# Attention on one core: a threshold on GpSimd, sums of even groups put elsewhere, weight parts made earlier

## The reference

```python
scores = (q @ k.T) / sqrt(64)
thresh = max(scores, -1) - tau
scores = where(scores >= thresh, scores, -1e9)
attn = exp(scores - max(scores, -1))
attn = attn / (sum(attn, -1) + 1e-9)
x = attn @ v                                   # then heads side by side: 2304 x 512
h = x @ w_in; sm = softmax(h); solu = h * sm
ln = (solu - mean) / sqrt(var + 1e-6) * g_ln; x = ln @ w_out
h = x @ w_in2; out = softplus(h) @ w_out2
```

## Time and profile before

| | |
|---|---|
| median of 3 runs | 910.83 us |
| the profiled execution | 911.15 us, span from first to last instruction 909.4 us |
| PE, DVE busy share of the span | 96%, 84% |
| ACT, POOL busy share of the span | 55%, 48% |
| chain that ended last | DVE 53%, PE 35%, issue 8% |
| attention | from 5.4 us (first score product) to about 254 us (last mask) |
| mean granted TensorE clock | 0.994 of full speed |

### The profile page before, as it was taken

The page is one execution under the profiler, slowest core; times in us unless marked ns, Lnnn a source line. Parts: engine busy times, 40 slices in busy tenths (PEclk is TensorE's granted clock), DMA queues, the critical chain, the costliest instruction groups (busy, mean ns, idle before and its releaser), DMA issues.

```text
span 909.4 us, 16546 instructions
## 1 busy us (share of the span) xinstructions
PE 869.7 (96%) x6104; PEld 726.3 (80%) x6104; DVE 762.1 (84%) x1376; ACT 501.7 (55%) x936; POOL 433.4 (48%) x449
## 2 busy tenths in 40 slices
PE   6899999999989999999998998999999999999997
PEld 4566666666667889889898897999989999899995
DVE  6999999999929754835641999999999999999997
ACT  4777877888846442433442564545545455455543
POOL 3445444447617612313311565565555556556563
PEclk9999999999999999999999899999999999999999
DMA  6813431342100000000002610000000000000000
GB/s 163 217 32 80 102 97 37 80 105 75 48 25 23 24 1 1 1 1 1 1 12 88 197 30 0 36 1 1 35 1 1 35 1 1 35 0 0 35 0 35
DMA packets 29496, 37.65 MB, mean 41 GB/s; under 512 B 3696, under 2 KB 17520, under 8 KB 29424
## 3 DMA queue, kind: packets, MB, share of 16 engines
q1 hardware_dynamic: 29024, 36.42, 14.5%
q10 hardware_dynamic: 400, 0.30, 0.1%
HBM read 31.98 MB, written 4.72 MB: 40 GB/s over the span
## 4 chain that ended last, share of the span: by engine, by line
DVE 53%; PE 35%; issue 8%; POOL 1%; ACT 1%; DMA 0%; ACTq 0%; DVEq 0%; POOLq 0%
DVE g L850 12%; PE y_ps L1044 11%; DVE ntop L710 8%; PE s_ps L942 7%; DVE g_hi L854 7%; DVE g L840 5%; PE h_ps L911 5%; DVE g_lo L856 5%; DVE g L843 5%; PE o_ps L982 4%; PE f_ps L1101 3%; PE m_ps L1020 2%; DVE x_lo L705 2%; DVE solu L807 1%; DVE st_top L793 1%
## 5 line engine op out<-in xcount | busy, mean ns | idle before, releaser
L451 POOL TENSOR_TENSOR w_lo<-w_raw,w_hi 128x512 fp32r<-128x512 f32 x96 | 129.6, 1351 | 163.6 <-ACT w_hi L632 163.6
L412 POOL TENSOR_SCALAR kept<-kept,inv 128x576 f32<-128x576 f32 x144 | 106.1, 756 | 117.9 <-DVE inv L742 117.8
L511 ACT ACTIVATE expd<-s_ps,ntop 128x576 f32<-128x576 f32 x144 | 106.3, 741 | 51.7 <-DVE ntop L710 51.7
L1020 PE MATMUL m_ps<-y_hi,w_lo 128*128 128x384 f32 x384 | 131.4, 342 | 0.0
L648 ACT ACTIVATE l<-u 128x384 f32<-128x384 f32 x96 | 50.4, 525 | 145.8 <-POOL u L459 145.8
L1020 PE MATMUL m_ps<-y_lo,w_hi 128*128 128x384 f32 x384 | 130.3, 339 | 0.0
L1020 PE MATMUL m_ps<-y_hi,w_hi 128*128 128x384 f32 x384 | 129.2, 336 | 0.0
L459 POOL TENSOR_TENSOR u<-z,consts 128x384 f32<-128x384 f32 x96 | 108.2, 1127 | 41.8 <-ACT z L641 41.7
L850 DVE TENSOR_TENSOR g<-g,l 128x384 f32<-128x384 f32 x96 | 125.7, 1309 | 2.7
L1101 PE MATMUL f_ps<-w_hi,g_hi 128*128 128x512 f32 x288 | 115.4, 401 | 8.9 <-DVE g_lo L856 8.9
L710 DVE TENSOR_REDUCE ntop<-s_ps 128x1 f32<-128x576 f32 x144 | 107.5, 757 | 14.2 <-PE s_ps L942 6.8
(11 more groups left out here) (87 smaller groups left out, 1815.1 us busy)
## 6 DMA issues: line engine op xcount, KB each, us to landing
q_sb<-q_t SPq DMA_DIRECT2D x28, 288.0 KB, 5.1
v_sb<-v_main SPq DMA_DIRECT2D x16, 256.0 KB, 3.2
stage<-w_in SPq DMA_DIRECT2D x16, 256.0 KB, 2.7
w_raw<-w_out SPq DMA_DIRECT2D x8, 512.0 KB, 4.8
out<-o_sb SPq DMA_DIRECT2D x5, 768.0 KB, 3.5
k_sb<-k_t SPq DMA_DIRECT2D x21, 144.0 KB, 4.4
stage<-w_in SPq DMA_DIRECT2D x4, 512.0 KB, 8.9
stage<-w_out SPq DMA_DIRECT2D x4, 512.0 KB, 3.7
```

The source lines that it names most:

```text
L412: nc.gpsimd.tensor_scalar(kept[:, tile % RING, :], kept[:, tile % RING, :], inv[:, group % 2, k:k + 1], 1.0, ALU.mult, ALU.mult).then_inc( ...
L451: nc.gpsimd.tensor_tensor(w4[1][:, n % 2, :], w4_raw[:, n % F2, :], f32(w4[0][:, n % 2, :]), ALU.subtract).then_inc(w4lo_made, 1)
L511: nc.scalar.activation(expd[:, tile % 2, :].rearrange("p (a b) -> p a b", a=2), s_ps[tile % 2][:, :, 0:HALF], ACT.Exp, bias=ntop[:, tile % ...
L1020: last = nc.tensor.matmul(m_ps[n % 4][:, 0:GC], w[:, k, (n % F2) * P:(n % F2 + 1) * P], y[odd][:, k, :], start=(k == 0 and m == 0), stop=( ...
```

## The change

GpSimd gets a loop over doubles instead of groups. In double u it makes the threshold of tile b (`make_threshold_b`), then the probabilities of the groups that ended in double u - 1, in the eighth double of a unit the key scalings of the next two pairs, and in doubles 28, 31, 37 and 40 two low parts each of the first matrix. VectorE makes the threshold of tile a alone; the semaphore is split in two. `raise_sums` of an even group moves from between the two maxima of the next double to behind the mask of b in the same double; odd groups stay. ScalarE's high parts go from doubles 54 to 61 to doubles 24 to 34, two in three.

```diff
+W1_LOW = (28, 31, 37, 40)
-        thresh_made = sem("thresh_made")
+        thresh_a, thresh_b = sem("thresh_a"), sem("thresh_b")
+        def complete(u):
+            return [group for group in range(GROUPS) if (GROUP * group + GROUP - 1) // 2 == u]
...
-            for group in range(GROUPS):
+            def make_threshold_b(u):
+                pool.wait_ge(top_made, 2 * u + 2)
+                col = slice((2 * u + 1) % 4, (2 * u + 1) % 4 + 1)
+                nc.gpsimd.tensor_scalar(thresh[:, col], ntop[:, col], -1.0, tau_sb[:, 0:1], ALU.mult, ALU.subtract
+                                        ).then_inc(thresh_b, 1)
+            def probabilities(group):
                 pool.wait_ge(inv_made, group + 1)
...
-                pair = 2 * ((group - 1) // 6 + 1) + (group - 1) % 6
-                if group > 0 and (group - 1) % 6 < 2 and pair < PAIRS:
-                    pool.wait_ge(k_in[pair % 4], 16 * len(k_pieces(pair)) * (pair // 4 + 1))
-                if 38 <= group < 38 + 2 * C:
-                    w1_low(group - 38)
+            pool.wait_ge(tau_in, 16)
+            for u in range(DOUBLES + 1):
+                if u < DOUBLES:
+                    make_threshold_b(u)
+                for group in complete(u - 1):
+                    probabilities(group)
+                unit, step = divmod(u, PT)
+                if step == PT - 2 and unit + 1 < UNITS:
+                    scale_keys(2 * unit + 2)
+                    scale_keys(2 * unit + 3)
+                if u in W1_LOW:
+                    for m in range(2):
+                        w1_low(2 * W1_LOW.index(u) + m)
...
-                if 54 <= v < 54 + 2 * C:
-                    w1_high(v - 54)
+                if 24 <= v < 24 + 3 * C and v % 3 < 2:
+                    w1_high(2 * (v // 3 - 8) + v % 3)
...
-                dve.wait_ge(thresh_made, tile + 1)
+                dve.wait_ge((thresh_a, thresh_b)[tile % 2], tile // 2 + 1)
...
-                for group in done:
-                    raise_sums(group)
-                if a < TILES:
+                for group in complete(u - 1):
+                    if group % 2 == 1:
+                        raise_sums(group)
+                if u < DOUBLES:
                     maximum(b)
-                    make_threshold(a)
-                    make_threshold(b)
-                for group in done:
+                    make_threshold_a(u)
+                for group in complete(u - 1):
                     invert(group)
-                if a < TILES:
+                if u < DOUBLES:
                     keep(a)
                     keep(b)
+                for group in complete(u):
+                    if group % 2 == 0:
+                        raise_sums(group)
```

More of the change, by code:

```diff
@@ L409, in _ @@
                 pool.wait_ge(inv_made, group + 1)
-                for k in range(GROUP):
-                    tile = GROUP * group + k
+                for tile in range(GROUP * group, GROUP * group + GROUP):
                     nc.gpsimd.tensor_scalar(kept[:, tile % RING, :], kept[:, tile % RING, :],
-                                            inv[:, group % 2, k:k + 1], 1.0, ALU.mult, ALU.mult
+                                            inv[:, group % 2, tile % GROUP:tile % GROUP + 1], 1.0, ALU.mult, ALU.mult
@@ L414, in _ @@
                                             ).then_inc(probs_made, 1)
-                pair = 2 * ((group - 1) // 6 + 1) + (group - 1) % 6
-                if group > 0 and (group - 1) % 6 < 2 and pair < PAIRS:
-                    pool.wait_ge(k_in[pair % 4], 16 * len(k_pieces(pair)) * (pair // 4 + 1))
-                    nc.gpsimd.tensor_scalar(k_sb[:, pair % 4, :, :], k_sb[:, pair % 4, :, :], 1.0 / 8, 1.0,
-                                            ALU.mult, ALU.mult).then_inc(k_scaled, 1)
@@ L421, in _, with scale_keys @@
-                if 38 <= group < 38 + 2 * C:
-                    w1_low(group - 38)
+            def scale_keys(pair):
+                pool.wait_ge(k_in[pair % 4], 16 * len(k_pieces(pair)) * (pair // 4 + 1))
+                nc.gpsimd.tensor_scalar(k_sb[:, pair % 4, :, :], k_sb[:, pair % 4, :, :], 1.0 / 8, 1.0,
+                                        ALU.mult, ALU.mult).then_inc(k_scaled, 1)
+            pool.wait_ge(tau_in, 16)
[11 more added lines that the diff above has]
+                        w1_low(2 * W1_LOW.index(u) + m)
@@ L711, in maximum, with make_threshold_a @@
                                         op=ALU.max, negate=True).then_inc(top_made, 1)
-            def make_threshold(tile):
-                col = slice(tile % 4, tile % 4 + 1)
-                dve.wait_ge(top_made, tile + 1)
+            def make_threshold_a(u):
+                col = slice(2 * u % 4, 2 * u % 4 + 1)
+                dve.wait_ge(top_made, 2 * u + 1)
                 nc.vector.tensor_scalar(thresh[:, col], ntop[:, col], -1.0, tau_sb[:, 0:1], ALU.mult, ALU.subtract
-                                        ).then_inc(thresh_made, 1)
+                                        ).then_inc(thresh_a, 1)
             def keep(tile):
                 dve.wait_ge(exp_made, tile + 1)
-                dve.wait_ge(thresh_made, tile + 1)
+                dve.wait_ge((thresh_a, thresh_b)[tile % 2], tile // 2 + 1)
                 wait(dve, left_made, (tile - RING) // 2 + 1)
@@ L745, in _ @@
                 a, b = 2 * u, 2 * u + 1
-                done = [group for group in range(GROUPS) if (GROUP * group + 2) // 2 == u - 1]
-                if a < TILES:
+                if u < DOUBLES:
                     maximum(a)
-                for group in done:
-                    raise_sums(group)
-                if a < TILES:
+                for group in complete(u - 1):
+                    if group % 2 == 1:
+                        raise_sums(group)
+                if u < DOUBLES:
                     maximum(b)
-                    make_threshold(a)
-                    make_threshold(b)
-                for group in done:
+                    make_threshold_a(u)
+                for group in complete(u - 1):
                     invert(group)
-                if a < TILES:
+                if u < DOUBLES:
                     keep(a)
                     keep(b)
+                for group in complete(u):
+                    if group % 2 == 0:
+                        raise_sums(group)
                 if u in (68, 69):
```

## The result

The changed kernel took 914.88 us (median of 10 runs, 910.78 to 915.00) against 910.68 us for the kernel before (10 runs, 907.11 to 912.03). The ratio is 1.0040, with a 95% interval of 1.0022 to 1.0057: 2.0 to 5.2 us slower. The profiled execution after took 914.90 us, with a span of 913.2 us.

A forecast was written before the change was run, and what follows sets the result against it. The prediction took the attention to be paced by a ring of VectorE and TensorE waiting on each other. Against 911.15 us profiled, -1.9 + 4.1 + 0.5 + 0 + 0 = +2.7 gave 913.85, median about 913.5, range 910.9 to 915.6.

The forecast's parts named there:

- the forecast itself: Whole kernel: the stall at the start, small savings and nothing else, 912 to 914.7 us; chance 0.63.
- a costlier stall: Rival, at the start: TensorE's clock falls for two doubles and masks follow late, 915.4 us; chance 0.15.
- Part 2, the stall: Double 0: threshold b waits on GpSimd behind key scalings, so the second mask is 4.1 us late, once.
- Part 3, the clock: TensorE, idle during the stall at the start, falls to 1.2 GHz: 0.5 us lost, bounds 0 to 1.6.
- Part 1, the small gain: Threshold b leaves VectorE: first mask 0.04 us earlier in 47 doubles with a group, 1.9 us gained.
- GpSimd's threshold: Threshold b on GpSimd takes 0.19 us, ready 0.4 us after the second maximum, covered before the second mask.
- Parts 4 and 5: Moved sums of even groups, and moved first-matrix parts and key scalings: all covered, 0 us each.
- The faster rival: VectorE bound by instruction time, not latency: each double loses threshold b's time, 901 to 905 us; chance 0.08.

The follow-up runs named there:

- e1: The kernel before with only threshold b of double 0 made on GpSimd, behind the four key scalings; 915.84 us, ratio 1.0049.
- e2: The changed kernel with the scaling of the second images' keys put behind threshold b of doubles 0 and 1; 907.77 us, ratio 0.9962.
- e3: The changed kernel with 30 dummy transposes on TensorE between the scores of the two tiles of double 1; 913.54 us, ratio 1.0030.
- e4: The kernel before with only the sums of even groups put behind the second mask; 910.45 us, ratio 0.9992.
- e5: The kernel before with only the first matrix's high and low parts and the later key scalings moved as in the change; 910.19 us, ratio 0.9995.
- e7: e2 with threshold a also made on GpSimd and the low parts made one per double; 904.04 us, ratio 0.9929.
- e9: e7 leaving out one of the ten products with the values per result, so not the whole computation; 897.70 us, ratio 0.9848.
- e6: The changed kernel with threshold b given back to VectorE, right behind threshold a; 910.00 us, ratio 1.0001.
- e8: e2 with threshold a moved on VectorE from behind the maximum of b to between the two maxima; 908.77 us, ratio 0.9974.

## Why the prediction was right, point by point

It was right in the sign and in the cause: 913.5 us in a range of 910.9 to 915.6, against 914.88. The size has some luck in it. 914.88 lies 0.2 us above the band of the forecast itself (912 to 914.7), in the part that was given to a costlier stall; neither of that rival's terms came (a threshold of 1.02 us, a clock cost of 1.6).

- **Part 2, the stall: right.** Predicted 13.71 us for the second mask of double 0 and 4.1 us lost; measured 13.66 and 4.06, once, with nothing that absorbs it (e1), and gone when the keys' scalings stand behind (e2). That the start came out to 0.05 us is luck, for two errors offset each other there (see the threshold below).
- **Part 3, the clock: right in the trace after.** 0.5 us was taken, 0.58 measured (e3). The same stall in e1 met the longer stretch and cost 1.24 us, inside the 0 to 1.6 that was given. Which of the two an execution gets was not foreseen.
- **Part 1, the small gain: right in mechanism, too large in size.** 0.04 us for 47 doubles, 1.9 us, was predicted; 1.5 was measured at the last mask. The mask moved up from 0.13 to 0.09 us behind threshold a, but the second mask follows the first by 0.743 us instead of 0.736 (medians of the doubles with a group, after and before), which takes a part back. Where the saving shows was wrong: not in both doubles with a group and nowhere else, but in the first of them and in the double without one.
- **GpSimd's threshold: right that it is covered, wrong in price.** 0.29 us, and 0.32 the first time, and not 0.19; the mask keeps 0.56 us to spare. At the start the threshold took 0.13 us longer than predicted but began 0.19 us earlier (13.24 against 13.35 + 0.08): the last scaling ended 0.11 us sooner in this trace, and no 0.08 us lay between the two.
- **Parts 4 and 5: right.** e4 and e5 measured zero for both.
- **The faster rival** (VectorE bound by its instruction time) is refuted by e2, which has all of its premise and gains 1.5 us where it asks for 10 to 14. e7 shows what it had seen rightly: there was time to win on VectorE, but it lay in how late threshold a is made and handed on, which the change left in place.
- **The sum's own shortfall.** Predicted +2.7 us, measured +3.2 at the softplus and 2.0 to 5.2 over the whole. Of the 0.5 us at the softplus 0.4 is part 1 and 0.1 the clock. What the last dense pair adds (0.6 us in the profiled executions) was not in the sum, and the forecast had said that nothing more would be lost behind the attention. The medians differ by 4.2 us; the 0.4 us beyond the 3.8 of the profiled spans is within the spread of the runs.

## What to carry to other kernels

When a step moves to another engine, read that engine's stream from its first instruction: a wait that was harmless with nothing urgent behind it becomes the kernel's wait, even if it lasts a few microseconds and occurs once. In a ring of short dependent steps, look at what the gap between an instruction's end and its dependent's start contains: an instruction issued inside a latency (threshold b in the doubles without a group) is free, and taking it away gives nothing, while starting the latency earlier (threshold a in e7) gains until the next thing shows behind it: here ScalarE's exponentials, and in every third double TensorE's own work (e9).

## What the runs showed of the hardware

- A 128x1 tensor_scalar with a scalar from SBUF takes 0.29 us on GpSimd and 0.20 on VectorE. The 128x1 tensor_tensor on which the prediction leaned (L432) takes 0.19. The longer one of rows 9, L429, has 18 pieces in the trace before: 0.19 us in the six that run while VectorE is idle, and 1.02 to 1.06 us in 11 of the 12 that overlap VectorE's product of two SBUF tensors (0.27 in the other). None of the 72 thresholds on GpSimd took more than 0.32 us in the trace after.
- The granted clock of TensorE fell to 1.2 GHz within an idle time of 3.84 us in the changed kernel, 0.20 us before its end, and stayed there for 3.41 us. In e1 it fell 1.57 us before the end of an idle time of 3.98 us and stayed for 6.82 us. With dummy transposes in the idle time it did not fall.
- The time of one and the same kernel spreads over some 6 us (906.45 to 912.71 in 23 runs of the kernel before). The profiled executions place much of it in the last dense pair, from the softplus's first instruction to the span's end: 413.5 us before, 414.1 after, 410.7 in e3. The trace of e3 has one stretch at half clock there:

```profile
503.15:506.57 3.42, 3.16 (x8) 2.52 (x9) 3.39 (x5) 2.23 (x5) 2.34 (x2) 0.50 1.10 354
507.00:909.00 402.00, 393.69 (x1960) 354.27 (x1958) 385.44 (x503) 203.72 (x388) 228.53 (x187) 1.00 0.06 22
```

  Before had 6.8 and 3.4 us, after four stretches (above). The eleven traces agree in order, by the time at half clock behind the softplus's first instruction: 410.7 us with 3.4 (e3), 412.0 and 412.2 with 8.0 and 6.8 (e5, e4), 412.8 to 413.5 with 10.2 to 11.1 (before, e1, e2, e6), 414.0 to 414.4 with 14.6 to 14.8 (after, e7, e8, e9). No edit tried it, and it is not all of the spread. Of the 23 runs, the four with a mean clock of 0.992 took 911.81 to 912.13 us and six of the eight with 0.998 took 906.45 to 909.64, but the other two took 912.25 and 912.71, which the clock does not explain. For a gain of 1 or 2 us in the attention, the shift of an event behind it says more than the median.
